# Linear attention before a channel-mixing block and a gated convolution: the key-value sums move from plain f32 products of twenty narrow matmuls to f32r products of split keys and a split v

## The chip, the cores and the metric

The kernel runs on one core of a Trainium2 chip. The metric is the device time of one execution in microseconds (us); the text gives the median of the runs shown. Engines are named as in the profile: PE is TensorE's matmul side, PEld its weight loads, DVE is VectorE, ACT is ScalarE, POOL is GpSimd, SP is the engine that issues the DMAs here.

## The reference, cut to what matters

```python
# q, k, v: (8 batches, 8 heads, 576 tokens, 64); w_phi: (64, 128)
def phi(x):
    proj = einsum('bhsd,df->bhsf', x, w_phi)
    proj = proj - max(abs(proj), axis=-1, keepdims=True)
    return concatenate([exp(proj), exp(-proj)], axis=-1)
q_p, k_p = phi(q), phi(k)
kv  = einsum('bhsf,bhsd->bhfd', k_p, v)
z   = sum(k_p, axis=2)
num = einsum('bhsf,bhfd->bhsd', q_p, kv)
den = einsum('bhsf,bhf->bhs', q_p, z)[..., None] + 1e-06
x   = heads_side_by_side(num / den)                 # (8, 576, 512)
# moe: a shift-mixed block, w_k 512x1024, w_v 1024x512, w_r 512x512
k = maximum(xk @ w_k, 0); v = k * k @ w_v
x = sigmoid(xr @ w_r) * v          # xk, xr: mixtures of x and x one token earlier
# moe2: h = relu(x @ w_in); 3-tap convolution over tokens; (h * sigmoid(conv)) @ w_out
```

All inputs and outputs are float32.

## The kernel before, in words

The program has two phases. Phase 1 does attention and the first block for all 8 batches, phase 2 the second block. The change touches phase 1 alone.

Phase 1 runs as a software pipeline: `work(None, (None, 0), ...)` does attention of batch 0 alone, seven iterations do the first block of batch c together with attention of batch c+1 (one written out, six in a loop), and a last one does the block of batch 7. Attention is done for two heads at a time, `PAIRS` = 4 pairs a batch. The order in which every engine meets the steps is a list that `iteration()` writes from a planner's figures: `PE_NS` says how long TensorE is taken to need for a step, `FILL_NS` how many ns of block tiles are put behind an attention step. All engines walk the same list and each does its own part of a step, strictly in that order, so a step that stands ahead in the list also stands ahead in every engine's queue.

A block tile is a `K`, `R` or `V` step: 12 matmuls of 128x288 (`V` has 24, cut into the steps `V-` and `V`), each operand split into a high and a low f32r part, three products for one (`three()`). `K-` and `K+` are the first nine and the last three matmuls of a K tile. Behind a K tile ACT does three operations (relu, the square rounded to f32r as high part, the square in f32) and DVE one (`tile_k`: the low part of the square). Behind an R tile ACT does the gate, behind a V tile DVE multiplies. K, R and V tiles rotate through three PSUM banks.

The attention steps of one pair before:
- `QP`: q times w_phi with tokens on partitions, DVE takes the maximum over features (`max_q`) and splits it. `KP`: the same for k, and DVE subtracts the maximum (`shift_k`).
- `M`: PE turns the split maxima into rows, ACT copies them. `P0`, `P1`: q's features with features on partitions, minus the maxima, in two halves of 288 tokens; ACT takes both exponentials (`exp_q`).
- `EK`: ACT takes exp(k) and exp(-k) (`exp_k`), two operations of 1280 elements.
- `KV`: `sum_kv`, 20 matmuls in plain f32: stationary an exponential of 128 tokens x 128 features, moving v with a column of ones, 65 columns. The column of ones gives z.
- `DEN`, `NUM`: denominators and numerators, 8 matmuls each; ACT copies both out. `RC`: DVE inverts the denominators that DMAs spread over partitions. `DV`: DVE multiplies, which gives x.

`XK`, `XR` are the shift-mixing of x on DVE, `HK`, `HR` the high parts on ACT, `LK`, `LR` the low parts on DVE, with n = 2 standing for the first half of the next batch; group 0 is pairs 0 to 2 and group 1 pair 3. In a steady iteration the list around pair 2 before is `V-03 EK2 P02 V03 DV1 K10 KV2 P12 K11 K12 DEN2 NUM2` (the numbers behind a tile's letter are half and index).

## Time and profile before

| | us |
|---|---|
| median of 3 runs | 1417.46 |
| the runs | 1412.54 to 1421.47 |
| profiled execution, its own time | 1417.62 |
| its span in the trace | 1415.8 |
| phase 1 (first matmul of phase 2 at) | 991.7 |
| attention of batch 0 alone (first block tile at) | 94.4 |
| one steady iteration | 118.0 |
| PE busy, share of the span | 96% |
| DVE busy / ACT busy | 672.6 / 626.6 |

The share of PE says that little of the span passes without a matmul under way. It is an average: in attention of batch 0 PE is busy 67 of 94 us, in a steady iteration 116 of 118.

### The profile page before, as it was taken

What the parts mean: (1) busy time and instruction counts of PE and PEld (TensorE: products, weight loads), DVE (VectorE), ACT (ScalarE), POOL (GpSimd) and SP (SyncE); (2) the same over time, 40 slices, a digit from 0 to 9 for tenths busy, and PEclk for the clock granted to TensorE, in tenths of its full rate; (3) what the DMA queues carried; (4) which work ended last, traced back from release to release, by engine and by line L of the source; (5) the groups of instructions that cost most, each with busy time, mean ns of one, the idle gap of its engine ahead of it and who ended that gap; (6) DMA issues with size and microseconds to landing.
All of it is one profiled execution on the core that took longest, in us unless ns stands there. A gap on an engine that the chain in (4) does not pass through costs nothing. (4 is left out here: it accounts for less than half of the span.)

```text
span 1415.8 us, 26326 instructions
## 1 busy us (share of the span) xinstructions
PE 1360.0 (96%) x10368; PEld 1211.6 (86%) x10368; DVE 672.6 (48%) x1047; ACT 626.6 (44%) x1111; POOL 13.5 (1%) x18
## 2 busy tenths in 40 slices
PE   5879999999999999999999999998899999999998
PEld 4668899889888889888988888998788988998997
DVE  5444244334433624442544362451757556655753
ACT  3536345454352534545445353443444443433532
POOL 0000000000000000000000000000300000000000
PEclk9879999999999999999999999999999999999999
DMA  5411202202212120220221212030310210110101
GB/s 165 124 45 40 58 27 77 63 20 69 61 45 70 40 58 26 62 78 19 70 54 53 69 41 58 25 116 22 93 64 1 71 64 30 41 63 30 41 30 38
DMA packets 94579, 78.60 MB, mean 56 GB/s; under 512 B 64656, under 2 KB 72976, under 8 KB 93456
## 3 DMA queue, kind: packets, MB, share of 16 engines
q1 hardware_dynamic: 94480, 77.10, 18.2%
q8 instruction: 84, 1.38, 0.4%
q14 instruction: 15, 0.12, 0.0%
HBM read 57.75 MB, written 19.02 MB: 54 GB/s over the span
## 5 line engine op out<-in xcount | busy, mean ns | idle before, releaser
L472 PE MATMUL psm<-xk_hi,wk_hi 128*128 128x288 f32 x512 | 158.6, 310 | 15.1 <-issue 6.9
L969 PE MATMUL psh<-y_hi,win_hi 128*128 128x288 f32 x512 | 153.9, 301 | 13.4 <-ACT h L1054 9.0
L818 DVE TENSOR_TENSOR k_lo<-square,k_hi 128x288 fp32r<-128x288 f32 x128 | 58.7, 458 | 221.3 <-ACT square L683 221.3
L472 PE MATMUL psm<-k_hi,wv_hi 128*128 128x288 f32 x512 | 154.4, 302 | 0.0
L472 PE MATMUL psm<-xk_lo,wk_hi 128*128 128x288 f32 x512 | 153.7, 300 | 0.0
L472 PE MATMUL psm<-xk_hi,wk_lo 128*128 128x288 f32 x512 | 153.2, 299 | 0.0
L970 PE MATMUL psh<-y_lo,win_hi 128*128 128x288 f32 x512 | 152.2, 297 | 0.0
L971 PE MATMUL psh<-y_hi,win_lo 128*128 128x288 f32 x512 | 151.6, 296 | 0.0
L472 PE MATMUL psm<-k_lo,wv_hi 128*128 128x288 f32 x512 | 151.1, 295 | 0.0
L472 PE MATMUL psm<-k_hi,wv_lo 128*128 128x288 f32 x512 | 150.8, 295 | 0.0
L1112 DVE SCALAR_TENSOR_TENSOR conv<-h,taps,conv 128x576 f32<-128x576 f32 x64 | 55.2, 863 | 141.3 <-ACT conv L1056 141.3
L472 PEld LDWEIGHTS psm<-xk_hi,wk_hi 128*128 128x128 f32 x512 | 98.8, 193 | 24.3 <-issue 16.3
L969 PEld LDWEIGHTS psh<-y_hi,win_hi 128*128 128x128 f32 x512 | 97.2, 190 | 16.2 <-ACT h L1054 11.3
L472 PE MATMUL ps<-q_exp,kvz 128*64 128x288 f32 (+1 forms) x992 | 102.1, 409 | 0.5 <-ACT q_exp L657 0.5
L472 PEld LDWEIGHTS psm<-k_hi,wv_hi 128*128 128x128 f32 x512 | 96.3, 188 | 6.6 <-issue 5.8
L678 ACT ACTIVATE relu<-psm 128x288 f32<-128x288 f32 x128 | 51.7, 404 | 113.4 <-PE psm L472 113.4
L971 PE MATMUL pso<-wout_hi,g_lo 128*128 128x512 f32 x256 | 101.1, 395 | 0.0
L969 PE MATMUL pso<-wout_hi,g_hi 128*128 128x512 f32 x256 | 101.0, 395 | 0.0
L970 PE MATMUL pso<-wout_lo,g_hi 128*128 128x512 f32 x256 | 101.0, 394 | 0.0
L1054 ACT ACTIVATE h<-psh 128x576 f32<-128x576 f32 x64 | 41.8, 653 | 129.4 <-DVE gated L1100 94.3
L472 PEld LDWEIGHTS psm<-xk_hi,wk_lo 128*128 128x128 f32 x512 | 98.9, 193 | 0.0
L472 PEld LDWEIGHTS psm<-xk_lo,wk_hi 128*128 128x128 f32 x512 | 98.8, 193 | 0.0
(116 smaller groups left out, 2810.9 us busy)
## 6 DMA issues: line engine op xcount, KB each, us to landing
v_nat<-in_v SPq DMA_DIRECT2D x32, 320.0 KB, 3.6
qk<-in_q SPq DMA_DIRECT2D x32, 288.0 KB, 2.9
qk<-in_k SPq DMA_DIRECT2D x32, 288.0 KB, 3.2
den<-den_scr SPq DMA_DIRECT2D x64, 144.0 KB, 3.0
y_scr<-y SPq DMA_DIRECT2D x64, 144.0 KB, 1.8
y<-y_scr SPq DMA_DIRECT2D x8, 1152.0 KB, 5.5
out<-rows SPq DMA_DIRECT2D x32, 256.0 KB, 2.0
den_parts<-den_rows SPq DMA_DIRECT2D x128, 2.2 KB, 1.9
```

What stands on the lines that cost most here:

```text
L472: return nc.tensor.matmul(o, lhsT, rhs, start=first, stop=last)
L678: nc.scalar.activation(relu[:, i % 2, :], psm[:, UNIT["K", n, i] % 3, 0:HALF], ACT.Relu).then_inc(k_relu, 1)
L818: nc.vector.tensor_tensor(k2_lo[:, i, :], square[:, i % 2, :], k2_hi[:, i, :].bitcast(F32), ALU.subtract).then_inc(k2_lo_ready, 1)
L969: nc.tensor.matmul(o, wh, xh, start=first, stop=False, skip_group_check=True)
L970: nc.tensor.matmul(o, wh, xl, start=False, stop=False, skip_group_check=True)
L971: return nc.tensor.matmul(o, wl, xh, start=False, stop=last, skip_group_check=True)
L1054: nc.scalar.activation(two(h[:, j % 2, 1:1 + S]), psh[:, j % 2, :, 0:HALF], ACT.Relu, scale=0.5).then_inc(h_ready, 1)
L1112: nc.vector.scalar_tensor_tensor(out=conv[:, j % 2, :], in0=h[:, j % 2, 0:S], scalar=taps[:, 0, j:j + 1], in1=conv[:, j % 2, :], op0=ALU.m ...
```

## The change

Per pair the steps become `E M EK PICK L0 KV0 L1 KV1 DEN NUM`.
- `E` (`features_and_keys`): k's projection with tokens on partitions as in `KP`, and q's features with features on partitions for all 576 tokens at once, which `P0` and `P1` did in halves; `QP` goes.
- DVE (`part_maxima`) finds q's maxima from the features: two 32x32-block transposes of 576 columns, a reduction over 1152 elements, then one PE transpose (`M`) and a small reduction. Four DMAs (`load_maxima`, issued by SP) lay the split maxima out as rows; `PICK` subtracts them.
- Each exponential of k is made twice on ACT, once rounded to f32r (`k_hi`) and once in f32; DVE subtracts (`low_keys`, steps `L0` and `L1`, 1280 elements each). POOL splits v (`split_v`). `sum_kv` runs as `KV0` and `KV1`: 10 matmuls of 130 columns (high, ones and low part of v beside each other) and 10 of 66 columns each, in f32r. ACT copies 260 columns and DVE adds the product with v's low part (`add_kv`).
- The planner's figures are new, and so are the places of the steps in the list. The copies of DEN and NUM both follow NUM. Around pair 2 the list is now `V-03 E2 V03 RC1 K10 M2 K11 K12 DV1 EK2 PICK2 K13 L02 K14 KV02 L12 K15 KV12 K16 DEN2 NUM2 E3`, and behind the last pair of a batch it is `KV13 DEN3 NUM3 V11 V-12 V12 XK20 V-13 HK20 RC3 V13 LK20`, where before it was `DEN3 R11 NUM3 RC3 R12 XK20 HK20 LK20 XR20 R13 HR20 V-10 LR20 V10 DV3 XK21`.
- Attention of batch 0 no longer runs q's and k's projections of batch 1's first pair ahead.

```diff
-PE_NS = {"QP": 1100, "KP": 1100, "M": 550, "P0": 800, "P1": 800, "KV": 2240, "DEN": 1000, "NUM": 1950,
+PE_NS = {"E": 2800, "M": 150, "PICK": 700, "KV0": 1300, "KV1": 1300, "DEN": 1200, "NUM": 2200,
-FILL_NS = {"QP": 2200, "M": 1600, "P0": 3500, "P1": 2600}
+FILL_NS = {"E": 3200, "M": 3200, "PICK": 1600, "L0": 1600, "L1": 1600, "KV1": 1200, "NUM": 1500}
...
+    def split_v(p, a):
+        await_(pool, v_loaded, 16 * PAIRS, a, 16 * (p + 1))
+        await_(pool, kv_summed, 2 * PAIRS, a, 2 * p)
+        nc.gpsimd.tensor_tensor(v_parts[:, :, :, 0:D], v_nat[:], ones[:].unsqueeze(2).unsqueeze(3).to_broadcast([P, TT, 2, D]),
+                                ALU.mult).then_inc(v_hi_ready, 1)
+        await_(pool, v_hi_ready, PAIRS, a, p + 1)
+        nc.gpsimd.tensor_tensor(v_parts[:, :, :, VLO:VP], v_nat[:], v_parts[:, :, :, 0:D].bitcast(F32), ALU.subtract).then_inc(v_ready, 1)
...
-    def sum_kv(p, a):
-        for e, src in enumerate((k_exp, k_shift)):
-            await_(pe, k_exp_ready, 2 * PAIRS, a, 2 * p + e + 1)
-            for h in range(2):
-                for t in range(TT):
-                    last = mm(ps[:, VW * (2 * h + e):VW * (2 * h + e) + VW], src[:, h, t, :], v_nat[:, t, h, :],
-                              t == 0, t == TT - 1)
+    def sum_kv(e, p, a):
+        await_(pe, v_ready, PAIRS, a, p + 1)
+        await_(pe, k_hi_ready, 2 * PAIRS, a, 2 * p + e + 1)
+        await_(pe, k_lo_ready, 2 * PAIRS, a, 2 * p + e + 1)
+        for h in range(2):
+            for t in range(TT):
+                mm(ps1[:, h, VP * e:VP * e + VP], k_hi[e][:, h, t, :], v_parts[:, t, h, :], t == 0, False)
+                last = mm(ps1[:, h, VP * e:VP * e + VLO], k_lo[e][:, h, t, :], v_parts[:, t, h, 0:VLO], False, t == TT - 1)
...
     def exp_k(p, a):
...
+        nc.scalar.activation(k_hi[0][:], k_shift[:], ACT.Exp).then_inc(k_hi_ready, 1)
+        nc.scalar.activation(k_exp[:], k_shift[:], ACT.Exp).then_inc(k_exp_ready, 1)
+        nc.scalar.activation(k_hi[1][:], k_shift[:], ACT.Exp, scale=-1.0).then_inc(k_hi_ready, 1)
+        nc.scalar.activation(k_shift[:], k_shift[:], ACT.Exp, scale=-1.0).then_inc(k_exp_ready, 1)
...
+    def low_keys(e, p, a):
+        await_(dve, k_exp_ready, 2 * PAIRS, a, 2 * p + e + 1)
+        await_(dve, k_hi_ready, 2 * PAIRS, a, 2 * p + e + 1)
+        await_(dve, kv_summed, 2 * PAIRS, a, 2 * p)
+        nc.vector.tensor_tensor(k_lo[e][:], (k_exp, k_shift)[e][:], k_hi[e][:].bitcast(F32), ALU.subtract).then_inc(k_lo_ready, 1)
```

On DVE, around pair 2 of a steady iteration, before. Here k2_lo is the low part of a K tile's square, and every such row waits for ACT's square of that tile.

```order
L756 TENSOR_REDUCE q_max<-ps0 128x10
L761 CAST q_max_split<-q_max 128x2x5
L763 TENSOR_TENSOR q_max_split<-q_max,q_max_split 128x2x5
L818 TENSOR_TENSOR k2_lo<-square,k2_hi 128x288
L777 SCALAR_TENSOR_TENSOR den_cols<-den_parts 128x9
L780 RECIPROCAL den_cols<-den_cols 128x9
L767 TENSOR_REDUCE k_max<-ps0 128x10
L771 TENSOR_TENSOR k_shift<-ps0,k_max 128x1280
L818 TENSOR_TENSOR k2_lo<-square,k2_hi 128x288 x2
L785 TENSOR_TENSOR x<-num,den 128x576
```

The same place on DVE now, from the split of q's maxima on. The rows k_lo0 and k_lo1 are the new low parts of the keys, for which the matmuls of KV0 and KV1 wait.

```order
L794 TENSOR_TENSOR q_max_split<-q_max,q_max_split 36x32
L798 TENSOR_TENSOR k_shift<-ps0,k_max 128x2x128
L801 TENSOR_TENSOR k_shift<-ps1,k_max 128x2x512
L858 TENSOR_TENSOR k2_lo<-square,k2_hi 128x288 x2
L825 TENSOR_TENSOR x<-num,den 128x576
L858 TENSOR_TENSOR k2_lo<-square,k2_hi 128x288
L808 TENSOR_TENSOR k_lo0<-k_exp,k_hi0 128x1280
L858 TENSOR_TENSOR k2_lo<-square,k2_hi 128x288
L808 TENSOR_TENSOR k_lo1<-k_shift,k_hi1 128x1280
```

Before, nothing for the key sums came from DVE behind k_shift. Now k_lo0 stands behind the k2_lo of the K tile that follows PICK, and k_lo1 behind that of the tile after it.

On ACT at the same place, before:

```order
L649 ACTIVATE k_exp<-k_shift 128x1280
L651 ACTIVATE k_shift<-k_shift 128x1280
L657 ACTIVATE q_exp<-ps1 128x2x288 x2
L678 ACTIVATE relu<-psm 128x288
L681 ACTIVATE k2_hi<-relu 128x288
L683 ACTIVATE square<-relu 128x288
```

And now:

```order
L670 ACTIVATE k_hi0<-k_shift 128x1280
L671 ACTIVATE k_exp<-k_shift 128x1280
L672 ACTIVATE k_hi1<-k_shift 128x1280
L674 ACTIVATE k_shift<-k_shift 128x1280
L681 ACTIVATE q_exp<-ps0 128x576 x4
L701 ACTIVATE relu<-psm 128x288
L704 ACTIVATE k2_hi<-relu 128x288
L706 ACTIVATE square<-relu 128x288
```

The square on which the k2_lo ahead of k_lo0 waits now stands behind four exponentials of k and four of q; before it stood behind two and two.

## Rows read from the trace of the kernel before

**Rows 1.** The page's first section, and PE's, PEld's, DVE's and ACT's busy time by stretch.

```profile
PE 1360.0 (96%) x10368; PEld 1211.6 (86%) x10368; DVE 672.6 (48%) x1047; ACT 626.6 (44%) x1111; POOL 13.5 (1%) x18
...
0.00:94.00 94.00, 66.55 (x556) 53.23 (x556) 45.74 (x56) 40.34 (x52) 2.63 (x14) 0.87 0.38 113
424.00:542.00 118.00, 115.90 (x978) 102.36 (x978) 48.17 (x83) 53.15 (x100) 0.00 (x0) 0.99 0.19 53
```

**Rows 2.** ACT's copies of one pair's numerators, one iteration apart: start, duration.

```profile
506.08 0.65 ACT L673 ACTIVATE num<-ps 128x576 f32<-128x576 f32 x1 [1.34 <-PE ps L472]
...
624.10 0.65 ACT L673 ACTIVATE num<-ps 128x576 f32<-128x576 f32 x1 [1.34 <-PE ps L472]
```

**Rows 3.** PE in order of time, one pair of a steady iteration.

```profile
502.79 3.24 PE L472 MATMUL ps<-q_exp,kvz 128*1 128x288 f32 x32
505.96 1.39 PE L472 MATMUL ps<-phi,qk 64*128 64x128 f32 x20
507.28 0.40 PE L472 MATMUL psm<-k_hi,wv_hi 128*128 128x288 f32 x1
507.52 0.29 PE L472 MATMUL psm<-k_lo,wv_hi 128*128 128x288 f32 x1
507.65 0.29 PE L472 MATMUL psm<-k_hi,wv_lo 128*128 128x288 f32 x1
...
510.38 0.74 PE L503 MATMUL ps<-ident,q_max_split 128*66 128x128 f32 x5
510.87 0.38 PE L472 MATMUL psm<-k_hi,wv_hi 128*128 128x288 f32 x1
...
512.63 0.76 PE L472 MATMUL ps<-qk,phi 64*128 64x288 f32 x4
513.45 0.40 PE L472 MATMUL psm<-k_hi,wv_hi 128*128 128x288 f32 x1
...
516.73 2.34 PE L472 MATMUL ps<-v_nat,k_exp 128*128 128x65 f32 x20
518.90 2.40 PE L472 MATMUL ps<-v_nat,k_shift 128*128 128x65 f32 x20
521.23 0.76 PE L472 MATMUL ps<-qk,phi 64*128 64x288 f32 x4
```

**Rows 4.** Groups by form: weight loads of 128 columns in f32r and in f32.

```profile
L472 PEld LDWEIGHTS psm<-k_hi,wv_hi 128*128 128x128 f32 x512 | 96.3, 188 | 6.6 <-issue 5.8
...
L472 PEld LDWEIGHTS ps<-v_nat,k_exp 128*128 128x128 f32 x600 | 69.8, 192 | 1.3 <-issue 1.3
```

**Rows 5.** ACT and then DVE in order of time, around pair 2's exponentials.

```profile
536.74 1.28 ACT L649 ACTIVATE k_exp<-k_shift 128x1280 f32<-128x1280 f32 x1 [0.15 <-DVE k_shift L771]
...
539.22 1.17 ACT L657 ACTIVATE q_exp<-ps 128x576 f32<-128x576 f32 x2
...
541.08 0.43 ACT L683 ACTIVATE square<-relu 128x288 f32<-128x288 f32 x1
...
541.54 0.46 DVE L818 TENSOR_TENSOR k_lo<-square,k_hi 128x288 fp32r<-128x288 f32 x1 [4.46 <-ACT square L683]
```

**Rows 6.** Groups by form on DVE: a reduction from PSUM, subtractions in SBUF, the product that gives x.

```profile
L756 DVE TENSOR_REDUCE q_max<-ps 128x10 f32<-128x1280 f32 x30 | 44.7, 1490 | 92.9 <-PE ps L472 92.9
...
L785 DVE TENSOR_TENSOR x<-num,den 128x576 f32<-128x576 f32 x32 | 24.1, 754 | 7.0 <-DMA den<-den_scr 7.0
...
L813 DVE TENSOR_TENSOR xk_lo<-mix,xk_hi 128x864 fp32r<-128x864 f32 x16 | 16.9, 1058 | 8.5 <-ACT xk_hi L694 8.5
```

**Rows 7.** Four small DMAs issued by SP one after the other: start of the first issue, time until the last has landed.

```profile
550.02 2.39 SPq L383 DMA_DIRECT2D den_parts<-den_rows  x4
```

**Rows 8.** PE's first matmul and first block matmul; the stretch behind it, granted clock 0.50.

```profile
6.04 2.50 PE L472 MATMUL ps<-phi,qk 64*128 64x128 f32 x20 [6.04 <-DMA phi<-in_w_phi]
...
94.37 0.58 PE L472 MATMUL psm<-xk_hi,wk_hi 128*128 128x288 f32 x1 [4.46 <-DVE xk_lo L813]
...
...
94.40:100.20 5.80, 5.80 (x24) 5.80 (x25) 2.71 (x6) 0.93 (x1) 0.00 (x0) 0.50 0.44 105
```

More of the change, by code:

```diff
@@ L48, in attention_steps @@
 def attention_steps():
-    steps = [("QP", 0)]
-    for p in range(PAIRS):
-        steps += [(s, p) for s in ("KP", "M", "EK", "P0", "KV", "P1", "DEN", "NUM")]
-        steps += [("QP", p + 1)] if p + 1 < PAIRS else []
-    return steps
+    return [(s, p) for p in range(PAIRS) for s in ("E", "M", "EK", "PICK", "L0", "KV0", "L1", "KV1", "DEN", "NUM")]
 def first_attention_steps():
-    steps = [("QP", 0), ("KP", 0)]
+    steps = [("E", 0)]
     for p in range(PAIRS):
         last = p == PAIRS - 1
-        def ahead(s):
-            return [(s, 0, "next") if last else (s, p + 1)]
         def before(s):
             return [(s, p - 1)] if p else []
-        steps += [("M", p)] + before("RC") + [("P0", p), ("EK", p)] + ahead("QP")
-        steps += [("KV", p), ("P1", p)] + before("DV") + ahead("KP") + [("DEN", p), ("NUM", p)]
+        steps += [("M", p)] + before("RC") + [("EK", p), ("PICK", p), ("L0", p), ("KV0", p), ("L1", p), ("KV1", p)] + before("DV")
+        steps += [] if last else [("E", p + 1)]
+        steps += [("DEN", p), ("NUM", p)]
         if last:
@@ L123, in iteration @@
             s, p = step[:2]
-            if not (ran_ahead and step in (("QP", 0), ("KP", 0))):
-                emit(step)
+            emit(step)
             if with_moe:
                 fill(FILL_NS.get(s, 0))
-                if s == "DEN":
+                if s == "NUM":
                     later += [(now + RC_AFTER, ("RC", p)), (now + DV_AFTER, ("DV", p))]
                     later.sort(key=lambda t: t[0])
-                if (s, p) == ("DEN", PAIRS - 1):
-                    fill(LAST_FILL)
         if with_moe:
@@ L344, in batches @@
         work((None, LAST), None, iteration(True, False))
-    def attention_of(step, a):
-        return (None, 1) if step[-1] == "next" else a
     block = ctx.enter_context(nc.Block())
@@ L375, in load_piece, with load_maxima @@
             sp.dma_start(dst, src[P * i:P * (i + rows), :].rearrange("(r p) n -> p r n", p=P)).then_inc(piece_loaded[n % 2], 16)
+        def load_maxima(p, a):
+            await_(sp, q_max_split_ready, PAIRS, a, p + 1)
+            await_(sp, features, PAIRS, a, p)
+            for h in range(2):
+                for part in range(2):
+                    row = 2 * h + part
+                    sp.dma_start(max_rows[row:row + 1, :].bitcast(F32), q_max_split[TOK * h:TOK * h + TOK, part, :].bitcast(F32)).then_inc(rows_loaded, 16)
         def spread_den(p, a):
@@ L394, in work @@
         def work(m, a, steps):
-            if a is not None and not second_of(a):
+            if a is not None:
                 load_qk(0, a)
@@ L407, in work @@
                 load_piece(1)
-            if a is not None and second_of(a):
-                load_qk(1, a)
             pieces = 2
@@ L471, in mm @@
         def mm(o, lhsT, rhs, first, last):
-            return nc.tensor.matmul(o, lhsT, rhs, start=first, stop=last)
+            return nc.tensor.matmul(o, lhsT, rhs, start=first, stop=last, skip_group_check=True)
         def three(o, w_parts, x_parts, first, last):
@@ new lines, in turn_maxima, with subtract_maxima @@
+        def turn_maxima(p, a):
+            await_(pe, q_part_ready, PAIRS, a, p + 1)
+            nc.tensor.matmul(turned_max(p, a), q_part[:], ident[:], start=False, stop=True, is_transpose=True,
+                             skip_group_check=True).then_inc(max_turned, 1)
+        def subtract_maxima(p, a):
+            await_(pe, rows_loaded, 64 * PAIRS, a, 64 * (p + 1))
+            await_(pe, k_tail_shifted, PAIRS, a, p + 1)
+            for h in range(2):
+                for chunk in CHUNKS[h]:
+                    cols = slice(*chunk)
+                    last = mm(q_cols(h, p, a)[:, cols], pick[:, h, :], max_rows[:, cols], False, True)
+            last.then_inc(features, 1)
@@ L672, in copy_num @@
             await_(act, x_ready, PAIRS, a, p)
-            nc.scalar.activation(two(num[:]), halves(ps1[:]), ACT.Copy).then_inc(num_copied, 1)
+            nc.scalar.activation(num[:], q_cols(0, p, a), ACT.Copy).then_inc(num_copied, 1)
         def tile_k(n, i, m):
@@ L728, in work @@
                     split_mix(int(kind == "HR"), step[1], step[2], (None, -1) if m is None else m)
-                if m is None and kind in ("QP", "KP", "P1") and pieces < len(PIECES):
+                if m is None and kind in ("M", "KV0", "NUM") and pieces < len(PIECES):
                     split_piece(pieces)
@@ L858, in work @@
                     tile_v(step[1], step[2], m)
-                if m is None and kind in ("QP", "KP", "P1") and pieces < len(PIECES):
+                if m is None and kind in ("M", "KV0", "NUM") and pieces < len(PIECES):
                     split_piece(pieces)
```

353 lines of the change are left out of this document (186 added, 167 removed).

## Prediction

> **What bounds the kernel now.** I read the page's first section first, then busy time by stretch [rows 1]. PE is busy 1360.0 of 1415.8 us, and 115.90 of 118.00 us in the stretch that is one steady iteration, since the same copy of numerators recurs after 624.10 - 506.08 = 118.0 us [rows 2]. There are seven such iterations, 826 us in all. DVE and ACT are busy 48 and 53 us of the 118. So PE bounds the iterations. Only work taken off PE shortens them, and only a wait that PE does not have today lengthens them. Attention of batch 0 is another matter: PE is busy 67 of 94 us there, and the chain through the engines sets the time.
>
> **PE's work, before.** Then I read PE in order of time [rows 3] and took each step from one start to the next. DEN and NUM 505.96 - 502.79 = 3.17 us; a projection (QP or KP) 1.32; M 0.49; a half of q's features with its maxima 0.82, two of them 1.64; KV 521.23 - 516.73 = 4.50. The pair has 3.17 + 2.64 + 0.49 + 1.64 + 4.50 = 12.4 us. A block matmul of 288 columns takes 0.13 us, and the first behind an attention step 0.24, so a tile of twelve takes 1.6 to 1.7.
>
> **KV, the centre of the change.** KV is 40 rows of 65 columns in 4.50 us, 112 ns each [rows 3]. A f32 product shows as two rows (10 products, 20 rows), a f32r product as one. So 20 f32 products become 40 f32r products: 40 rows of matmul before and 40 after, each with its own load of 128 weight columns. The question is what sets the 112 ns. In f32r 288 columns stream in 132 ns, so 65 columns would be 30 ns in one pass and 60 in two; the streaming is not what costs 112 ns. The weight loads are 128 columns wide in both formats and last 188 ns in f32r and 192 in f32 [rows 4], alike. I conclude that 112 ns is the pace of weight loads and that f32r does not change it: streaming 130 columns (60 ns) and 66 columns (30 ns) stays hidden under it. KV0 and KV1 together come to 40 x 0.112 = 4.5 us: no gain. Bounds from rows: if f32r loads were hidden, 20 x 0.060 + 20 x 0.030 = 1.8 us; if narrow f32r matmuls were four times slower per column than the wide ones, 20 x 0.24 + 20 x 0.12 = 7.2 us. No row has a f32r matmul under 288 columns. I take 4.5, since both kinds of load read the same.
>
> By the Trainium skill, "FP8 and Floating Point Precision", section "TensorE Precision Notes", true f32 makes four passes through the array. Counted so, a token tile streams 4 x 65 = 260 columns before and 130 + 66 = 196 after, which would make KV a quarter shorter, 1.1 us a pair. The trace speaks against counting columns here, because 65 columns in two rows take 224 ns.
>
> **The rest of PE's work.** E: the k projections stay 1.32. The features are 576 columns for each of two heads in f32. P0 and P1 had the two heads beside each other in the array's halves (0.82 with the subtraction). E orders a 512-column piece of one head, then small ones, then the 512-column piece of the other, so the two hardly overlap; DEN and NUM show the price of a f32 row of 288 columns: DEN has 16 rows in four column groups side by side, NUM 16 in two, so 3.17 us are 4 + 8 rows' time, 0.26 us for one and 0.92 ns a column. Two heads x 512 columns x 2 rows x 0.92 ns = 1.9 us, less the key tiles beside them: E is 2.8 to 3.2, I take 3.0. M is one transpose instead of five, 0.15. PICK is two times 576 f32r columns, 0.53 us of streaming, 0.7 with its start. DEN and NUM have the same columns, 3.2. Sum 3.0 + 0.15 + 0.7 + 4.5 + 3.2 = 11.6 us: **0.85 us less a pair, 3.4 us an iteration**. That alone would be 24 us over seven iterations.
>
> **ACT and DVE.** ACT gets two more exponentials of 1280 elements at 1.29 us and loses a copy. DVE per pair: a reduction of 1280 from PSUM is 1.49 us, a subtraction of 864 is 1.058, so about 1.04 ns an element and 0.15 us fixed [rows 6]. Two transposes of 576 have no row; between the 0.46 us of a 288-column subtraction [rows 5] and the 1.49 of the 1280-element reduction I take the 0.75 of the product of 576 columns, the nearest in size. Then a reduction of 256 (0.42), of 1152 (1.36), of 1024 (1.22), small ones of 0.6 together, shifts of 256 and 1024 (1.64), two low parts of 1280 (1.49 each), add_kv 0.42. Together 10 us a pair where it was 4.8. Both engines still have room: DVE rises to some 70 us in an iteration. Neither becomes the bound by its sum. What matters is the order.
>
> **The new waits, pair 2, worked out.** Take 0 as the end of E2 on PE. A PE result is usable 0.25 us after its place in the queue (a transpose group starts at 510.38, lasts 0.74, and the next starts at 510.87 [rows 3]).
> - DVE transposes to 1.75, tail reduction 2.2, large reduction 3.55; PE has V03 and K10 to do, 3.25 us. M at 3.6: PE waits 0.35.
> - On DVE behind it stand the reduction of k (4.8), V03's product (5.2), RC1 (5.6), K10's k2_lo (6.1), and only then the split of the maxima, 6.7. Four DMAs take 2.4 [rows 7], so the rows are there at 9.1. PE has K11 and K12 and is done at 7.0. PICK2 waits 2.2 us and ends at 9.9.
> - k_shift is ready at 8.4; ACT is free of K12 at 8.5. Four exponentials of k end at 13.7, four of q (two take 1.17 [rows 5]) at 16.0. K13 is done on PE at 11.6, but its relu, square and square come behind them on ACT: 17.3. The k2_lo of K13 on DVE is 17.7, and only behind it k_lo0, 19.2. PE has K13 and K14, done at 13.2. **KV02 waits 6.1 us** for DVE.
> - The same order of queues is seen in the trace of before: the square of the K tile behind P02 comes after two exponentials of k and two of q, and its k2_lo on DVE after 4.46 us of idle time (the profile writes k_lo for it) [rows 5]. It cost PE nothing because no matmul waited for DVE. Now KV does.
> - KV02 to 21.6, K15, KV12 to 25.5, K16, DEN and NUM to 30.3. E3 needs the features' banks, which hold the sums until ACT has made both copies (0.25 + 2 x 0.65): it waits 1.5.
>
> Pair 2 has 0.35 + 2.2 + 6.1 + 1.5 = 10.1 us of waiting.
>
> **The other pairs, in the same way.** Pair 0 has K tiles too: 2.2 at PICK and 6.3 at KV0. It also begins behind a worse tail. After NUM3 PE has five half V tiles, 8 us. The mixing XK20 stands on DVE behind V12's product (5.3), takes 1.05 + 1.4, then ACT's high part 0.93, then on DVE V13's product and the low part 1.06: about 10, so K-00 waits 2.0. Group 1 needs RC3, two chained DMA steps, DV3, and two more splits, to about 17.7 on DVE; E0's transposes stand behind that, and M0 waits 3.1. Pair 0: 13.6. Pair 1 is among V tiles, whose DVE part needs no ACT operation behind the exponentials: 2.8 at PICK, 0.5 at KV0. Pair 3: about 0.5 at KV0, and DEN3 directly behind KV13 waits 1.0 for the copy and add_kv. In all 10.1 + 13.6 + 3.3 + 1.5 = **28.5 us an iteration**.
>
> **The clock.** After 4.46 us of idle time PE ran 5.8 us at a granted clock of 0.50 (1.2 GHz), 24 matmuls at 0.24 us instead of 0.13 [rows 8]. KV has two waits of over 6 us an iteration. Behind each PE is the bound again, so about 5 us at half speed cost 2.5 each: 5 us an iteration, with 0 and 12 as ends (behind the smaller waits PE waits again anyway).
>
> **Attention of batch 0.** Here the chain from k_shift to k_shift is: four exponentials 5.15, k_lo1 1.5, KV1 2.4, copy and add 0.9, E 3.0 (it waits for add_kv), DEN and NUM 3.2, then DVE's 3.3 + 1.2 + 0.6 + 1.6 = 23 us a pair, against (94.4 - 6.0)/4 = 22 with start and tail in it [rows 8]. With E0 at 6.0 and at half clock the first k_shift is there at 18.6; + 3 x 23.4 + 10.2 to the fourth pair's add_kv + 3.2 + 3.6 for copies, high and low parts gives the first block tile at 106 instead of 94.4: +12 us. The last iteration and phase 2 do not change, and the memsets and POOL's splitting of v (a pair ahead of its use) are free.
>
> **The sum.** 7 x (28.5 - 3.4 + 5) + 12 = 211 + 12 = +223 us on 1417.6, the profiled execution's own time, which lies on the median (1417.5): **1640 us**.
>
> **Rivals.**
> - Cheap f32r loads. The planner's 1300 ns for a half of KV would be 65 ns a matmul. At the bound of 1.8 us for KV an iteration loses 10.8 us more work: 1640 - 76 = 1564, and with no clock loss 1530. Rows 4 speak against it. By the Trainium skill, "TensorE: Matmul & The Clock Gate", section "Weight-path perf modes — Fast Weight Load (FWL) and DoubleRow", the fast weight load is used for 128 weights when the type is not FP32, which f32r might count as; the 188 ns rows do not show it. Chance 0.15.
> - Dear narrow f32r matmuls, 7.2 us: + 2.7 x 28 = 76, 1716. Chance 0.1.
> - Faster: the waits are covered and only PE's sum counts, 1417.6 - 24 = 1394, or 1318 with cheap loads. It decides at waits under 3.4 us an iteration (14 with cheap loads). It would need k_lo0 not to wait for K13's square, and the lists of both engines say that it does. Chance 0.04. Near no change 0.03.
> - Waits about half my size, because PE's steps overlap better than added up: 7 x (14 - 3.4 + 2) + 12 = +100, 1518. Chance 0.1.
>
> My own case has 0.58. The range goes from 1530 to 1720. The noise of a measurement of this kernel is about 1%. Faster by over 1% 0.04, within 1% 0.03, slower 0.93.
>
> **What the profile after would show.** If right: PE's idle time before the first v_parts matmul of KV0 in pairs 0 and 2 is about 6 us, ended by DVE k_lo; an iteration is 140 to 155 us; 20 rows of v_parts matmuls in 2.1 to 2.4 us at the full clock; 0.50 of granted clock after the long waits; DVE's k_lo1280 rows right behind a k2_lo that waited for ACT's square. Wrong would be: v_parts matmuls at 50 to 70 ns each, KV0 waits under 2 us, PE idle mostly for rows_loaded or for E, or an iteration under 118 us.

## The result, and the profile after

The changed kernel takes **1739.31 us** (median of 4 runs, 1736.57 to 1747.2), the kernel before 1419.1 on the same chip (4 runs, 1412.54 to 1421.47): ratio 1.2275, 95% interval 1.2216 to 1.2333. That is 320 us slower where the prediction said 223, and above its range, which ended at 1720.

The profiled execution of after took 1738.44 us. First come the page's first line on the engines and busy time by stretch, one steady iteration and then attention of batch 0 (columns as in [rows 1]: length, busy time and count of PE, PEld, DVE, ACT, POOL, granted clock, DMA share, GB/s).

```profile
PE 1457.9 (84%) x9600; PEld 1305.1 (75%) x9600; DVE 834.0 (48%) x1303; ACT 677.4 (39%) x1143; POOL 107.0 (6%) x83
...
604.60:758.40 153.80, 126.06 (x902) 112.87 (x901) 70.38 (x116) 61.03 (x109) 11.55 (x8) 0.89 0.14 41
0.00:136.50 136.50, 75.49 (x420) 60.89 (x420) 60.46 (x83) 46.28 (x56) 14.89 (x23) 0.72 0.24 73
```

PE's first block matmul:

```profile
136.89 0.37 PE L495 MATMUL psm<-xk_hi,wk_hi 128*128 128x288 f32 x1 [3.29 <-DVE xk_lo L853]
```

The iteration went from 118.0 to 153.8 us, and the first block tile from 94.37 [rows 8] to 136.89. Phase 2 begins at 1310.75 where it began at 991.7, so all of the 320 us but 2 lies in phase 1: 42.5 in batch 0 and 277 behind it, in the iterations. Their lengths fall into two kinds, 153.7 to 154.0 and 157 to 158, the first one 165. The kinds differ by the clock and not by the waits: the iteration of 153.8 us above waits 27.7 us and loses 15.8 us to the clock, the one of 157.7 us ahead of it (446.8 to 604.5) waits 26.1 and loses 21.2.

For the clock I read the granted clock in stretches of 0.5 us and summed (1 - clock) x PE's busy time in each: the iteration of after loses 15.8 us to it. (Summed over all time, idle time too, it is 17.1; where the experiments give the "clock loss" of one iteration, it is that figure.) So the iteration splits into waits 27.7, clock 15.8 and what is left, 126.1 - 15.8 = 110.3 us of work at full clock. For the kernel before I take the iteration of [rows 2], from one copy of numerators to the next:

```profile
506.08:624.10 118.02, 116.56 (x998) 103.02 (x1000) 49.70 (x84) 54.83 (x105) 0.00 (x0) 1.00 0.19 53
```

It has waits 1.5, clock 0, work 116.5. (The stretch from 424 to 542 in [rows 1] is cut out of an iteration of 120.2 us, the one in which the clock drops once, for 1.7 us; hence its 0.99.) The change is +26.2 + 15.8 - 6.2 = +35.8 us.

What PE waited for in the steady part of after (us in all, times, longest):

```profile
PE ps L495 <- DMA max_rows<-q_max_split: 119.2, 28, 6.0
PE ps L495 <- DMA qk<-in_k: 26.0, 7, 6.8
PE ps L495 <- DVE k_lo L808: 18.9, 14, 2.0
PE psm L495 <- DVE xk_lo L853: 11.9, 6, 2.0
PE ps L495 <- ACT num L696: 10.1, 7, 1.5
PE ps L495 <- DVE kvz L812: 7.0, 7, 1.0
```

Most of it is the wait for the rows of the maxima ahead of PICK, 4.3 us in each pair. The wait for k_lo, which I had at 6 us for two pairs of each iteration, is 1 to 2. Pair 2 shows how the two hang together. PE, then the DMAs that SP issues, then DVE:

```profile
543.69 0.27 PE L541 MATMUL ps<-ident,q_part 128*128 128x128 f32 x1
551.96 1.65 PE L495 MATMUL ps<-max_rows,pick 128*128 128x512 f32 x4 [4.83 <-DMA max_rows<-q_max_split]
559.79 0.30 PE L495 MATMUL ps<-v_parts,k_hi 128*128 128x130 f32 x1 [0.76 <-DVE k_lo L808]
559.92 0.25 PE L495 MATMUL ps<-v_parts,k_lo 128*128 128x66 f32 x1
...
561.93 0.37 PE L495 MATMUL ps<-v_parts,k_lo 128*128 128x66 f32 x1
...
573.87 0.34 PE L495 MATMUL ps<-phi,qk 64*128 64x128 f32 x1 [1.48 <-ACT num L696]
```

```profile
545.09 0.42 SPq L399 DMA_DIRECT2D den_scr<-den_cols  x1
546.63 1.10 SPq L403 DMA_DIRECT2D den<-den_scr  x2
547.83 3.03 SPq L386 DMA_DIRECT2D max_rows<-q_max_split  x4
```

```profile
546.03 0.18 DVE L794 TENSOR_TENSOR q_max_split<-q_max,q_max_split 36x32 fp32r<-36x32 f32 x1
...
557.78 0.46 DVE L858 TENSOR_TENSOR k_lo<-square,k_hi 128x288 fp32r<-128x288 f32 x1 [6.98 <-ACT square L706]
558.15 1.49 DVE L808 TENSOR_TENSOR k_lo<-k_exp,k_hi 128x1280 fp32r<-128x1280 f32 x1
```

The split is ready at 546.21, but SP is in RC1: it waits for den_scr and issues the two loads of den at 546.63, and the rows' DMAs go out at 547.83, 1.6 us late. The four take 3.03 us from first issue to last landing, and PE starts 4.1 us after the first issue; I had 2.4 for the whole, from four DMAs of den_parts [rows 7]. Then the two tiles of K between PICK and KV0 run at half clock but for the last three matmuls, so that DVE's chain (the k2_lo that waits 6.98 us for ACT's square, then k_lo0, as drawn up) has nearly caught up when PE comes to KV0. From 559.79 to 561.93 are 19 steps from row to row, 113 ns each on average (0.14 us behind a row of 130 columns, 0.08 to 0.09 behind one of 66): the pace of before [rows 3].

### The profile page after: what moved, and what is told of

Same layout as the page of the kernel before. It is cut to its first block and busy times, and to the rows that moved or that the text cites. A ratio compares the mean times of both kernels' runs of the same rounds, so it can differ in the third digit from the quotient of the medians.

```text
span 1736.6 us, 25628 instructions
## 1 busy us (share of the span) xinstructions
PE 1457.9 (84%) x9600; PEld 1305.1 (75%) x9600; DVE 834.0 (48%) x1303; ACT 677.4 (39%) x1143; POOL 107.0 (6%) x83
## 5 line engine op out<-in xcount | busy, mean ns | idle before, releaser
L495 PE MATMUL ps<-v_parts,k_hi 128*128 128x130 f32 x640 | 176.0, 338 | 25.1 <-DVE k_lo L808 25.1
L495 PE MATMUL psm<-xk_hi,wk_hi 128*128 128x288 f32 x512 | 177.5, 347 | 19.7 <-DVE xk_lo L853 19.7
L495 PEld LDWEIGHTS ps<-v_parts,k_hi 128*128 128x128 f32 x640 | 145.5, 227 | 28.7 <-issue 28.7
L495 PE MATMUL ps<-v_parts,k_lo 128*128 128x66 f32 x640 | 167.0, 275 | 0.0
L1012 PE MATMUL psh<-y_hi,win_hi 128*128 128x288 f32 x512 | 154.7, 302 | 13.4 <-ACT h L1097 9.1
L495 PE MATMUL ps<-max_rows,pick 128*128 128x512 f32 (+1 forms) x120 | 46.4, 528 | 133.6 <-DMA max_rows<-q_max_split 133.6
L495 PEld LDWEIGHTS ps<-v_parts,k_lo 128*128 128x128 f32 x640 | 146.1, 228 | 0.2
L495 PEld LDWEIGHTS ps<-max_rows,pick 128*128 128x128 f32 x120 | 29.1, 299 | 143.5 <-DMA max_rows<-q_max_split 140.8
L495 PEld LDWEIGHTS psm<-xk_hi,wk_hi 128*128 128x128 f32 x512 | 117.0, 229 | 23.6 <-issue 19.6
L495 PEld LDWEIGHTS ps<-phi,qk 64*128 64x128 f32 x632 | 87.1, 227 | 52.8 <-issue 29.8
L495 PE MATMUL ps<-phi,qk 64*128 64x128 f32 x632 | 86.0, 329 | 43.4 <-DMA qk<-in_k 26.0
```

Source lines behind the costliest of these rows:

```text
L495: return nc.tensor.matmul(o, lhsT, rhs, start=first, stop=last, skip_group_check=True)
L1012: nc.tensor.matmul(o, wh, xh, start=first, stop=False, skip_group_check=True)
```

## The experiments

Times are medians; the kernel before took 1423.6, 1420.3, 1418.5 and 1419.5 in the four groups of runs, and each ratio is to that of its group. In the expectations a clock loss of an iteration is the figure over all time.

One iteration is a small sample, since in the changed kernel alone the clock loss goes from 17.1 to 22.2 from one to the next. So here is the same split for all of phase 1 behind batch 0, from the first block tile to the first matmul of phase 2, in us of the profiled execution: what PE waited, what the clock cost while PE was busy (in stretches of 0.5 us), and the rest, PE's work at full clock. It is one execution of each kernel, and the executions of one kernel differ by up to 30 us.

| kernel | length | waits | clock | work |
|---|---|---|---|---|
| before | 897 | 15 | 6 | 876 |
| after | 1174 | 203 | 135 | 836 |
| without the rows' DMAs | 1176 | 191 | 151 | 834 |
| tile behind L0 | 1109 | 186 | 86 | 837 |
| both | 1090 | 134 | 118 | 838 |
| rows' DMAs ahead on SP | 1198 | 203 | 156 | 838 |
| new order of tiles | 1237 | 207 | 194 | 836 |
| 30 matmuls ahead of PICK | 1152 | 122 | 80 | 951 |
| key sums in f32 | 1105 | 183 | 85 | 838 |
| 66 columns for 130 | 1201 | 207 | 160 | 834 |
| 260 columns for 130 | 1130 | 204 | 82 | 844 |
| 260 columns, tile behind L0 | 1113 | 182 | 90 | 841 |
| before, 40 f32r rows of 66 | 931 | 18 | 41 | 872 |
| before, 40 f32r rows of 132 | 897 | 17 | 3 | 877 |
| before, 20 f32r rows of 66 | 861 | 37 | 10 | 814 |
| before, 20 f32r rows of 132 | 861 | 38 | 8 | 815 |
| before, with a wait | 1141 | 102 | 166 | 872 |

The work hardly moves where no matmul was added or taken out, so what the edits change is waits and clock.

### The two waits of a pair

**Without the rows' DMAs.**

```diff
-                if kind == "M":
-                    load_maxima(step[1], a)
...
-            await_(pe, rows_loaded, 64 * PAIRS, a, 64 * (p + 1))
-            await_(dve, rows_loaded, 64 * PAIRS, a, 64 * p)
```

> The changed kernel without the four DMAs that lay q's split maxima out as rows, and without the waits for them; the rows stay zero, so the subtraction of q's maxima is left out of the result. Theory R (the rows' way through SP's queue and four DMAs is what PE waits for): the 16.7 us of waits at PICK in an iteration go, the clock recovers about 8 us more, attention of batch 0 gets about 30 us shorter; from 1739 to about 1540. Theory K (the prediction's: k_lo behind a K tile's square would bound as soon as the rows are in time): the waits go, but KV0's wait in pairs 0 and 2 grows from 0.8 to 2 us to 5 or 6; about 1600. If neither: above 1690.

Measured 1726.94 (ratio 1.2118, 1.1928 to 1.2308). The wait did not go, it moved:

```profile
PE ps L493 <- DVE k_lo L804: 121.0, 27, 7.5
PE ps L493 <- DMA qk<-in_k: 26.9, 7, 4.6
```

119 us for rows became 121 for k_lo: in a steady iteration 7.4 and 7.5 us in pairs 0 and 2, 1.8 and 0.6 in pairs 1 and 3, where I had worked out 6.3, 6.1, 0.5 and 0.5 ahead of KV0. So that wait exists; in the changed kernel the rows' wait hides it. Theory K's waits came out and neither theory's time: the two executions, 1716 and 1738, are not clearly shorter than the 1739 of after, and what the waits gave back (12 us) the clock took (16).

**The tile behind PICK moved behind L0**, so that k_lo0 no longer waits for that tile's square.

```diff
-FILL_NS = {..., "PICK": 1600, "L0": 1600, "L1": 1600, ...}
+FILL_NS = {..., "L0": 3200, "L1": 1600, ...}
```

> The changed kernel with the block tiles that stood between PICK and L0 put behind L0, so that k_lo0 on DVE no longer stands behind the low part of the K tile. PE's own order is the same. Theory R: little, since the rows bind; only the k_lo waits of 2.9 us an iteration go: 1715 to 1735. Theory K: if k_lo0 were a main cause, 6 us in each of two pairs: about 1650.

Measured 1670.89 (1.1725, 1.1638 to 1.1811), 68 us less. An iteration is 146.8 us, 7 less, with 120 us of waits for rows left and none for k_lo. Where one tile stands ahead of one subtraction is worth 68 us. The waits for k_lo were only 19 us in all; by the table waits give 17 us and the clock 49.

**Both.**

> Both edits together: no DMAs for the rows of maxima and no wait for them (the subtraction of q's maxima is left out of the result), and the block tiles behind PICK put behind L0. Theory B (two chains end close together in pairs 0 and 2, the rows' and k_lo0's behind the K tile; taking one away leaves the other): more than the sum of the two alone (-12 and -68 us), since nothing then stands in for the rows; an iteration of about 130 us, 1540 to 1580 in all. If the two were separate costs that add up: about 1660.

Measured 1652.45 (1.1641, 1.1574 to 1.1707). Theory B's 1540 to 1580 failed, and the sum of the two effects alone, about 1660, is what came. Taking out the rows' DMAs and moving one tile does not free PE: k_lo is still waited for, 62 us in all, and the loads of q and k 29 us; with the clock's 118 us these are most of what is left.

**The rows' DMAs issued ahead on SP**, right behind E's loads, so that RC does not hold them (in batch 0 a weight piece goes behind them too).

```diff
-                if kind == "M":
+                if kind == ("E" if m is not None else "M"):
                     load_maxima(step[1], a)
```

> The changed kernel with SP's queue in another order: in the iterations the DMAs for the rows of maxima are issued right behind the loads of E, ahead of RC's store and loads and of the V tile's store; in attention of batch 0 the weight piece of NUM is loaded behind them. Theory Q (SP's queue holds the rows up): they start 1.6 us earlier in pairs 1 and 2, 4 us earlier in two pairs of batch 0: 1715 to 1725 at most 15 us less in the iterations, because k_lo0 is next. Rival: no change (1735 to 1745), the issue time of the four DMAs being all of it.

Measured 1750.39 (1.233, 1.2169 to 1.2492): no gain, as the rival had it. The rows' waits fell from 119 to 85 us, k_lo's rose from 19 to 49.

**A new order of tiles**: three behind E, three behind M, none behind PICK, the order of SP above, and two of the four DMAs on ACT's queue.

```diff
-FILL_NS = {"E": 3200, "M": 3200, "PICK": 1600, "L0": 1600, "L1": 1600, "KV1": 1200, "NUM": 1500}
+FILL_NS = {"E": 4700, "M": 4700, "L0": 1600, "KV1": 1500, "NUM": 1500}
```

> An attempt at an order for the changed kernel: three block tiles behind E and three behind M, none behind PICK, one behind L0, KV1 and NUM; SP's queue as in the run on its order; two of the four DMAs for the rows issued by ACT. The result is complete. Expected if waits and clock are all of the loss: PE waits at PICK and KV0 under 1 us each; left are the batch's tail (about 8 us with the clock) and 3.4 us less work than before: 125 to 130 us an iteration, 1500 to 1550 in all. Rival: the waits move to the tail of the batch, since fewer tiles are left there: above 1600.

Measured 1804.23 (1.271, 1.2645 to 1.2775), the slowest of all. The rows' wait is gone (14 us in all), and k_lo's is 129, up to 6.8 at a time, at a mean clock of 0.848. Both expectations missed: the waits went neither away nor to the batch's tail. Work ahead of PICK covers the rows; what PE then lacks is work ahead of KV0.

**PE kept busy through the wait** by 30 further matmuls ahead of PICK.

```diff
         def subtract_maxima(p, a):
+            if not first_of(a):
+                await_(pe, k_shifted, PAIRS, a, p + 1)
+                for _ in range(30):
+                    mm(ps1[:, 0, 0:HALF], wk_hi[:, 0, 0:P], wk_hi[:, 1, 0:HALF], True, True)
```

> The changed kernel with 30 extra matmuls of 288 columns on PE before PICK, into the bank that k_main has left, so that PE is busy while it waits for the rows; outside batch 0. Their results are never read. Theory C (idle time costs twice, since the granted clock falls to 0.50 behind it): PICK and the next tiles run at full clock, about 8 of the 14 us that the clock costs an iteration come back: 1680 to 1700, though PE does 4 us more work a pair. Rival (the clock is no matter, or falls for another reason): 1739 or above, up to 1739 + 28 x 2.

Measured 1719.74 (1.2067, 1.1997 to 1.2138). The rows' wait is 1 us in all, and k_lo's 33 and k_shift's 24 took its place (the second is of the edit's own making: it makes PE wait for k_shift). By the table PE has 114 us more work, waits 81 us less and loses 55 us less to the clock, 7.9 an iteration, which is theory C's 8; its time of 1680 to 1700 was missed. So keeping PE busy gives clock back, but it costs nearly as much work as it saves; on the whole the added matmuls buy back 20 us.

### The key sums

**Key sums in f32 as before, all else changed.**

```diff
-                    mm(ps1[:, h, VP * e:VP * e + VP], k_hi[e][:, h, t, :], v_parts[:, t, h, :], t == 0, False)
-                    last = mm(ps1[:, h, VP * e:VP * e + VLO], k_lo[e][:, h, t, :], v_parts[:, t, h, 0:VLO], False, t == TT - 1)
+                    last = mm(ps1[:, h, VP * e:VP * e + VW], (k_exp, k_shift)[e][:, h, t, :], v_parts[:, t, h, 0:VW], t == 0, t == TT - 1)
```

> The changed kernel with the key-value sums in f32 again: 20 products of 65 columns on k_exp and k_shift, no k_hi and k_lo, no add_kv; all else stays. The result is complete. Theory W (128-column weight loads set the pace, f32 and f32r alike): KV stays 4.5 us a pair on PE, and what changes is the waits behind k_lo and add_kv, about 4 us an iteration, and 4 to 5 us a pair in attention of batch 0: about 1680. Rival (f32r is cheaper per product): the f32 sums cost PE up to 2.6 us a pair more, 28 x 2.6 = 73 us, so 1740 or above.

Measured 1659.59 (1.1645, 1.1584 to 1.1706), near theory W's 1680; the rival's 1740 falls. PE's work is the same in both formats, 838 and 836 us. So 80 of the 320 us hang on the f32r key sums with their two exponentials and low parts: by the table 50 of clock and 20 of waits, and 9 more in batch 0. The other 236 are there without them. What else is new there is the features' order, the maxima through DMAs, the one buffer for q and k and the order of tiles; their shares were not measured apart.

**k_hi's matmuls with 66 columns instead of 130.**

```diff
-                    mm(ps1[:, h, VP * e:VP * e + VP], k_hi[e][:, h, t, :], v_parts[:, t, h, :], t == 0, False)
+                    mm(ps1[:, h, VP * e:VP * e + VLO], k_hi[e][:, h, t, :], v_parts[:, t, h, 0:VLO], t == 0, False)
```

> The changed kernel with 66 columns instead of 130 in the matmuls of the keys' high part: the product with v's low part is left out of the result. Theory W (the load of 128 weight columns sets the pace of KV): 112 ns a matmul as before and no change, 1730 to 1745. Rival (streaming sets it): 64 columns less in 20 matmuls a pair, 30 ns each, 0.6 us a pair and 19 us in all.

Measured 1767.04 (1.2448, 1.2384 to 1.2511). Half the columns made the kernel 28 us slower, which neither theory held. By the table 25 of them are clock, and the work is no less. That led to the opposite edit.

**260 columns instead of 130.**

```diff
+                    mm(ps1[:, h, VP * e:VP * e + 2 * VP], k_hi[e][:, h, t, :], v_parts[:, t, :, :].rearrange("p h n -> p (h n)"), t == 0, False)
```

> The changed kernel, but each of the 20 k_hi matmuls of the key sums streams 260 columns (both heads' v parts) instead of 130. Changed in what is computed: the sums of the second head of a pair are made with the first head's v. Theory C (the granted clock, which falls in stretches where PE does little, took the 28 us that narrower matmuls had cost): 260 columns take about 0.12 us each, still at the pace of the weight loads, so the work hardly grows, and the clock loss of an iteration falls from 17 towards 12 us: about 1700, mean clock 0.90 or more. Rival N (the narrow version was slower for another reason, columns beyond 130 are only more work): 20 x 4 x 0.01 to 0.04 us more an iteration, 1740 to 1765, clock 0.89 or less.

Measured 1697.72 (1.1969, 1.1916 to 1.2021), as theory C had it: twice the columns, 41 us less. The waits are the same, the work is 8 us more, the clock costs 53 us less. Three widths stand in a row: 66 columns 1767, 130 columns 1739, 260 columns 1698.

**260 columns, and the tile behind L0.**

> The same 260 columns, and PICK's tile of filling moved behind L0 as in the run that gave 1671 (no wait for k_lo in the iterations). Changed in what is computed: the sums of the second head of a pair are made with the first head's v. Theory C: the two add up, 1671 - 35 = about 1635, clock 0.91 or more. Rival N: 1670 to 1695, clock 0.90 as there.

Measured 1678.92 (1.1833, 1.1789 to 1.1878): theory C's 1635 failed, the two don't add up. Without the k_lo wait the width no longer matters (1671 with 130 columns). Three different edits, the tile behind L0, 260 columns and the key sums in f32, each bring the clock's share from 135 us to 82 to 86, and two of them together not below that (90). Why isn't shown.

### In the kernel before, one thing at a time

The kernel before has one wait of 1.5 to 2.1 us in a steady iteration and the clock at full but for one dip of 1.7 us, so here each cost stands nearly alone.

**40 f32r rows of 66 columns for the 40 rows of f32.** `k_r` is the exponentials rounded by ACT, `v_r` is v rounded by POOL.

```diff
-                        last = mm(..., src[:, h, t, :], v_nat[:, t, h, :],
-                                  t == 0, t == TT - 1)
+                        for i in range(2):
+                            last = mm(..., src[:, h, t, :], v_r[:, t, h, :],
+                                      t == 0 and i == 0, t == TT - 1 and i == 1)
```

> The kernel before, with its key sums alone changed: ACT writes both exponentials of the keys rounded to f32r, POOL rounds v to f32r, and each of the 20 f32 products becomes two equal f32r matmuls of 66 columns (both kinds of sum are doubled, and the quotient stays). What is left out: the low parts of the keys and of v. 40 rows of PE before and 40 now, no new wait. Pace theory (40 rows at 112 ns, whatever the format): KV stays 4.5 us and the time 1415 to 1430, clock 0.98. Rival P (f32r loads alone are cheap, as the planner's 65 ns say): KV 2.6 us, 60 us less, 1360. Rival C (f32r matmuls this narrow lower the granted clock even where PE never waits): the profile's clock under 0.96 and 1440 to 1500.

Measured 1480.04 (1.0467, 1.0402 to 1.0532), 62 us slower without a new wait. PE in order of time, and the windows of one iteration, of the key sums and of the stretch right behind them:

```profile
421.52 0.29 PE L490 MATMUL psm<-xk_hi,wk_lo 128*128 128x288 f32 x1
421.65 4.55 PE L490 MATMUL ps<-v_r,k_r 128*128 128x66 f32 x40
426.13 1.33 PE L490 MATMUL ps<-qk,phi 64*128 64x288 f32 x4
```

```profile
411.00:534.00 123.00, 121.09 (x998) 106.77 (x1000) 50.58 (x84) 55.03 (x105) 5.82 (x4) 0.96 0.17 51
421.60:426.10 4.50, 4.50 (x42) 4.49 (x40) 0.46 (x1) 1.60 (x4) 0.00 (x0) 1.00 0.35 106
426.00:430.00 4.00, 4.00 (x19) 3.30 (x19) 0.00 (x0) 1.58 (x3) 1.25 (x1) 0.57 0.00 0
```

The key sums last 426.13 - 421.65 = 4.48 us, 112 ns a row: the same as in f32 [rows 3], so rival P falls and the pace theory's price for KV holds. But behind them the granted clock is down at 0.57 for 4 us while PE never stops, and so in three of the four pairs. The iteration is 123 us: 5 more, and the clock loss is 5.1. Seven times that and 10.8 us in batch 0 (first block tile at 105.13) are the 45 us by which the profiled span of 1460.9 exceeds that of before; the other executions were longer, up to 1494.

**The same with 132 columns in each row.**

```diff
-                            last = mm(ps[:, VW * (2 * h + e):VW * (2 * h + e) + VW], src[:, h, t, :], v_r[:, t, h, :],
+                            last = mm(ps[:, VW * (2 * h + e):VW * (2 * h + e) + 2 * VW], src[:, h, t, :], v_r[:, t, :, :].rearrange("p h n -> p (h n)"),
```

> The run in which the kernel before made its key sums by 40 f32r rows of 66 columns (1480, and 5.1 us of clock lost in an iteration), with 132 columns in each row. Changed in what is computed: the low parts of the keys and of v are left out, and a part of the sums is overwritten by the other head's. Theory C (narrow f32r rows cost clock and nothing else): the pace of 112 ns a row stays, the clock loss goes, 1420 to 1435, clock 0.97 or more. Rival (f32r rows behind 128-column loads cost clock at any width, or the rounding on POOL costs it): 1475 to 1490, clock 0.95.

```profile
433.60:551.40 117.80, 116.55 (x997) 103.00 (x997) 50.83 (x84) 54.86 (x104) 5.51 (x4) 1.00 0.18 53
```

Measured 1421.07 (1.0007, 0.9983 to 1.003): twice the columns, and all of the 62 us are back. The clock stands at 1.00 through the iteration. It was the narrow rows and nothing else of that edit: not the format, not the exponentials in f32r, not the rounding on POOL, which are all still there.

**Each product once** (`range(1)` for `range(2)`), 20 rows of 66 columns, and **once with 132**.

> As the run above with each product issued once: 20 f32r rows of 66 columns in place of 40 rows of f32. What is left out: the low parts of the keys and of v. Pace theory: KV 20 x 0.112 = 2.25 us a pair, 2.25 less, 9 us an iteration, 72 in all: 1348, clock 0.98. Rival C (less work, lower clock): 1380 or more, clock under 0.96.

> The run with 20 f32r rows of 66 columns in the kernel before (1380), with 132 columns in each. Changed in what is computed: as in the run above. Theory C: the clock lost with 66 columns comes back, 1350 to 1365. Rival: 1378 to 1385.

Measured 1380.38 (0.9746, 0.9703 to 0.979) and 1378.07 (0.9712, 0.9662 to 0.9761). Twenty rows less are 20 x 0.112 x 4 = 9.0 us an iteration by the pace theory; the iteration is 113.2 and 112.2 us. PE has become short of work, 4.1 and 4.4 us idle. Without idle time and clock an iteration is 107.5 and 107.8 us of work where it was 116.5: the 9 us are there, and a part of the gain is lost to waits. Of the expectations for 66 columns neither held whole: 1380 is rival C's time, but the clock is at 0.98 and an iteration loses 1.5 us to it, so 20 such rows hardly do what 40 do, and the width gives nothing (the rival of the second run). The first of the two computes the reference but for the low parts of the keys and of v, and it is faster than both kernels.

**A wait and nothing else.**

```diff
+                if kind == ("M" if m is None else "KV"):
+                    if m is not None:
+                        await_(sp, k_exp_ready, 2 * PAIRS, of, 2 * step[1] + 2)
+                    for i in range(4):
+                        sp.dma_start(hold[i:i + 1, :], ident[i:i + 1, :]).then_inc(held, 16)
...
             await_(pe, v_loaded, 16 * PAIRS, a, 16 * (p + 1))
+            await_(pe, held, 64 * PAIRS, a, 64 * (p + 1))
```

> The kernel before with nothing added but a wait: at each KV, SP issues four small DMAs of a constant once both exponentials of the keys are made, and PE waits for them ahead of the key sums (in attention of batch 0 they are issued earlier). The computation is whole. PE should wait some 3 to 4 us a pair, 12 to 16 an iteration. Theory W (waits cost clock besides: of the 17.1 us that an iteration of the changed kernel loses, 5.1 are the narrow rows' and 12 come with 27.7 us of waits, 0.43 per us): 118 + 14 + 6 = 138 an iteration, 1418 + 7 x 20 = about 1560, clock 0.94. Rival (waits of this length cost themselves alone): 118 + 14 = 132, about 1515, clock 0.98.

Measured 1685.86 (1.1877, 1.182 to 1.1934): 266 us for four small waits an iteration. One iteration and one stretch in it, and what PE waited for in that iteration:

```profile
383.80:536.20 152.40, 138.15 (x997) 121.86 (x998) 49.81 (x84) 55.05 (x105) 0.00 (x0) 0.85 0.15 41
...
455.80:466.80 11.00, 11.00 (x54) 10.22 (x54) 0.00 (x0) 1.58 (x3) 0.00 (x0) 0.53 0.13 29
```

```profile
PE ps L478 <- DMA hold<-ident: 12.1, 4, 3.7
PE psm L478 <- issue: 2.1, 1, 2.1
```

```profile
455.51 3.90 PE L478 MATMUL ps<-v_nat,k_exp 128*128 128x65 f32 x20 [3.68 <-DMA hold<-ident]
459.21 4.47 PE L478 MATMUL ps<-v_nat,k_shift 128*128 128x65 f32 x20
```

The 40 rows of key sums behind the wait take 8.1 us instead of 4.5, and the clock is back only 11 us later. In the iteration 14.2 us of waits brought a clock loss of 22.2: 14.2 - 1.5 (wait of before) + 22.2 = 34.9, against the 34.4 us by which it grew. Theory W was right in kind and much too low in size: not 0.43 us of clock for a us of waiting, but 1.6. Even the shortest of the four waits, 1.80 us in pair 3, has such a stretch behind it:

```profile
519.22 2.85 PE L478 MATMUL ps<-v_nat,k_exp 128*128 128x65 f32 x20 [1.80 <-DMA hold<-ident]
...
519.30:531.00 11.70, 11.70 (x62) 10.65 (x66) 0.60 (x2) 2.34 (x5) 0.00 (x0) 0.58 0.01 1
```

Each of these waits stands ahead of the 65-column rows of the key sums. Whether the same wait ahead of wide matmuls would cost as much was not tried. By the Trainium skill, "TensorE: Matmul & The Clock Gate", section "HAM oscillation — how this bites in real kernels", a DMA wait that comes back in each step lets the clock fall each time, so that every step starts slow. These rows agree in that; the 5.1 to 6.8 us of clock behind each wait are measured here.

## Why the prediction was wrong

The direction held, and so did the pace of the key sums; the size fell short by 97 us and the time lay 19 us above the range. The terms of the sum, in us of the profiled executions:

| term | forecast | measured |
|---|---|---|
| waits, seven iterations | 7 x 28.5 = +200 | +188 |
| work, seven iterations | 7 x -3.4 = -24 | -40 |
| clock, seven iterations | 7 x 5 = +35 | +129 |
| attention of batch 0 | +12 | +42.5 |
| phase 2 | 0 | +2 |
| all | +223 | +321 |

The clock and batch 0 were mis-sized; the other two were near and too high.

- **The pace of the key sums: right.** 112 ns a row; 113 were measured in after, 112 in the kernel before with f32r rows, of 66 columns and at the same time for 132. The rivals of cheap and dear f32r rows both fall (the factor of four in the dear one came from no row). That it is the weight loads which set this pace is argued, since no run had a narrower load. What I missed is that rows of equal duration aren't equal for the clock.
- **The waits of an iteration: right in sum by luck, wrong in place.** 28.5 forecast, 27.7 measured; but PICK has 16.7 where I had 7.2 in all, and the two KV steps 2.9 where I had 13.4, and the errors cancel. The step that failed is "Four DMAs take 2.4, PICK2 waits 2.2". The rows came 4.1 us after the first issue, and SP issued them 1.6 us after the split was ready, since I had counted RC1 on DVE and not on SP, where its loads wait for den_scr. PICK waits 4.1 to 4.8 us, in pair 3 3.0. The KV0 wait of 6.1 is then 0.8 to 1.7, that of pair 0 (6.3) 1.0 to 2.0; without the rows' DMAs they were there, 7.4 and 7.5.
- **A wait left out.** E0 waited 3.3 us for k: q and k have one buffer now, and SP issues q's load at 616.38 for an E0 that starts at 620.56, where before it was fetched a pair ahead. The line of the diff is `qk[:, 0, 0:S]`; I did not price it. It is 26 us in all.
- **PE's work: -6.2 us an iteration, forecast -3.4.** E took 2.77 us and not 3.0; for the rest no single step stands out.
- **The clock: the step that failed most.** The term "about 5 us at half speed cost 2.5 each: 5 us an iteration", with 12 as its upper end, was 15.8 in the iteration shown and 129 us over all seven, 18 each. I priced two long waits by one stretch of 5.8 us at 0.50 in rows 8 and took the small ones as free. The waiting experiment shows that waits of 1.8 to 3.7 us are not free at all (5.1 to 6.8 us of clock behind each), and the f32r rows add clock loss of their own. The term is 94 us too small, where 97 are missing in all; batch 0 was 30 us too small besides, and waits and work, 28 us lower than forecast, make up for that.
- **Batch 0: +42.5 us, forecast +12.** Three rows of pair 1 there and its window:

```profile
43.58 0.47 PE L541 MATMUL psm<-ident,q_part 128*128 128x128 f32 x1 [3.19 <-DVE q_part L781]
52.97 1.65 PE L495 MATMUL psm<-max_rows,pick 128*128 128x512 f32 x4 [8.91 <-DMA max_rows<-q_max_split]
60.68 0.45 PE L495 MATMUL ps<-v_parts,k_hi 128*128 128x130 f32 x1 [1.96 <-DVE k_lo L808]
```

```profile
34.00:67.50 33.50, 18.46 (x108) 15.15 (x106) 14.44 (x19) 11.55 (x14) 3.09 (x3) 0.64 0.26 84
```

```profile
45.82 0.38 SPq L377 DMA_DIRECT2D diff<-in_moe_w_v  x1
46.24 2.47 SPq L394 DMA_DIRECT2D den_parts<-den  x4
48.84 3.03 SPq L386 DMA_DIRECT2D max_rows<-q_max_split  x4
```

A pair takes 33.5 us there, not 23.4 (the steps that I listed add up to 22.9). I had priced the chain from k_shift to k_shift with PE's steps at full clock; they run at 0.64: KV1 takes 4.4 us for 2.4, E 4.6 for 3.0. And the chain lacked a piece. The fourth exponential of k ends at 52.85, but k_lo1 starts on DVE only at 59.05, 6.2 us later:

```profile
57.91 1.23 DVE L770 TENSOR_TENSOR wv_lo<-diff,wv_hi 128x1024 fp32r<-128x1024 f32 x1 [6.00 <-ACT wv_hi L663]
59.05 1.48 DVE L808 TENSOR_TENSOR k_lo<-k_shift,k_hi 128x1280 fp32r<-128x1280 f32 x1
```

Ahead of it stands the low part of a weight piece, which waits for ACT, and ACT first does q's exponentials, which wait for PICK. PICK waits 8.91 us for the rows: the split is ready at 46.41, but ahead of the rows on SP stand a load of weights and the four DMAs of den_parts. That wait looks like the cause and is not: in the run without the rows' DMAs it is gone, and the first block tile comes at 134.87, only 2 us earlier, because waits for k_shift (2.7) and k_lo (3.6 and 2.3) take its place in the pair.

What each cause, waits or narrow rows, holds of the clock's share can't be split cleanly, since the costs are not additive: 266 us for waits of 14 us an iteration in the kernel before, 62 for narrow rows, 320 for 28 us of waits with both. In after 203 us of waits lose less clock (135) than 102 do in the waiting experiment (166). What decides how long the clock stays down behind a given wait stays open.

## What to carry to other kernels

Where PE is at 96% and at full clock, price a new wait at its own length and again at what the clock loses behind it: here 13 us of added waits an iteration cost 34. Look for the wait behind the one you find: 119 us of waits for rows, taken away, came back as 121 us for k_lo, and moving a tile from behind PICK to behind L0 was worth more than taking four DMAs out. Judge the clock over all iterations and not by one. Of a step that uses DMAs, walk SP's queue as closely as DVE's. And where narrow rows follow each other at one pace whatever their width (112 ns here, with 65 to 132 columns), more columns are nearly free and may even give time back; with the k_lo wait gone they gave none.
